# An attention step in another order: transposes in two groups between the scores, the output matmuls right ahead of the weighing

## What is computed

```
q: (4, 8, 1152, 64); k, v the same             # batch, heads, sequence, head size
q_pool = q.reshape(B, H, 576, 2, 64).mean(axis=3)
scores = scale * q_pool @ k^T                   # 576 x 1152 for each of 32 heads
attn   = exp(scores - max) / (sum + 1e-9)
x      = attn @ v, heads side by side           # (4, 576, 512)
logits = x @ w_gate                             # 8 experts; a ninth column, w_local, says "stay with
                                                # the expert of the token before"
out    = p[e] * (relu(x @ w1[e]) @ w2[e])       # one expert e for each token, 512 -> 1024 -> 512
```

## Time and profile before

| | |
|---|---|
| median of 3 runs | 824.21 us (821.65 to 826.23) |
| profiled execution | 825.53 us, span 823.7 us |
| busy | TensorE matmuls 98%, VectorE 55%, ScalarE 53%, GpSimd 45% |
| granted TensorE clock | 0.994 of full speed |
| attention | up to about 504 us; routing and experts after it |
| two middle phases, 13 and 14 | 30.08 us (first transposes at 201.16 us and at 231.24 us) |

### The profile page before, as it was taken

One profiled execution on the slowest core, in us unless ns is written; L12 is line 12 of the kernel. 1 busy time (PEld: TensorE's weight loads), 2 busy tenths in 40 slices (PEclk: granted clock), 3 DMA queues, 4 the chain that ended last, 5 costly groups with the idle time before them and its releaser, 6 DMA issues.

```text
span 823.7 us, 14479 instructions
## 1 busy us (share of the span) xinstructions
PE 806.9 (98%) x5291; PEld 528.5 (64%) x5292; DVE 453.4 (55%) x644; ACT 440.5 (53%) x876; POOL 366.6 (45%) x357
## 2 busy tenths in 40 slices
PE   7999999999999999999999999999999999999997
PEld 6787887878878778788788676633433433433432
DVE  6876776766757767767777555622332332332321
ACT  4776765866866767767667662224324324324321
POOL 5875666656647657557567512021221221221221
PEclk8999999999999999999999999999999999999999
DMA  7433243243243333344561005976615375010010
GB/s 242 162 124 97 83 160 99 63 156 102 71 146 101 84 134 93 115 126 127 187 210 45 15 1 154 327 251 229 229 47 184 109 257 184 27 45 20 31 45 20
DMA packets 52549, 100.94 MB, mean 123 GB/s; under 512 B 25406, under 2 KB 25936, under 8 KB 52499
## 3 DMA queue, kind: packets, MB, share of 16 engines
q1 hardware_dynamic: 48931, 90.03, 33.9%
q0 software_dynamic: 3568, 10.23, 3.6%
HBM read 90.78 MB, written 9.99 MB: 122 GB/s over the span
## 4 chain that ended last, share of the span: by engine, by line
PE 94%; DVE 3%; ACT 1%; DMA 1%; issue 0%; POOL 0%; SPq 0%; POOLq 0%; DVEq 0%
PE psum L599 15%; PE psum L638 15%; PE psum L1458 15%; PE psum L1480 15%; PE psum L669 13%; PE psum L626 4%; PE psum L705 2%; PE psum L653 2%; PE psum L1470 2%; PE psum L687 2%; PE psum L1393 2%; PE psum L673 2%; PE psum L1384 2%; PE psum L1446 1%; DVE negmax L983 1%; ACT probs L776 1%
## 5 line engine op out<-in xcount | busy, mean ns | idle before, releaser
L983 DVE TENSOR_REDUCE negmax<-psum 128x1 f32<-128x1152 f32 x144 | 195.4, 1358 | 64.0 <-PE psum L599 45.1
L599 PE MATMUL psum<-kstack,qstack 128*128 128x384 f32 x756 | 165.3, 354 | 0.2
L638 PE MATMUL psum<-ident,probs 128*128 128x128 f32 x1152 | 160.6, 275 | 2.1 <-DVE oT L997 1.2
L768 ACT ACTIVATE pT<-psum 128x512 f32<-128x512 f32 x192 | 114.9, 598 | 58.8 <-PE psum L638 56.8
L638 PEld LDWEIGHTS psum<-ident,probs 128*128 128x128 f32 x1152 | 134.9, 141 | 16.0 <-issue 6.2
L599 PEld LDWEIGHTS psum<-kstack,qstack 128*128 128x128 f32 x756 | 127.7, 190 | 0.9 <-ACT probs L776 0.9
L1460 PE MATMUL psum<-second,xgT 128*64 128x512 f32 x288 | 127.6, 595 | 0.0
L1458 PE MATMUL psum<-wbuf,xgT 128*64 x288 | 127.5, 595 | 0.0
L1480 PE MATMUL psum<-wbuf,shared 128*64 x288 | 126.6, 592 | 0.0
L1482 PE MATMUL psum<-second,shared 128*64 128x512 f32 x288 | 126.6, 592 | 0.0
L776 ACT ACTIVATE probs<-psum,negmax 128x768 f32<-128x768 f32 x128 | 115.7, 904 | 17.8 <-DVE negmax L983 17.4
(11 more groups left out here) (261 smaller groups left out, 1032.7 us busy)
## 6 DMA issues: line engine op xcount, KB each, us to landing
wbuf<-in_w SPq DMA_DIRECT2D x64, 512.0 KB
kraw<-in_k_t SPq DMA_DIRECT2D x32, 576.0 KB, 4.1
qraw<-in_q_t SPq DMA_DIRECT2D x31, 576.0 KB, 3.9
vraw<-in_v_t SPq DMA_DIRECT2D x16, 576.0 KB, 4.0
x_rows<-x_out SPq DMA_DIRECT2D x32, 128.0 KB
second<-in_w SPq DMA_DIRECT2D x8, 512.0 KB, 6.1
x_rows<-x_out SPq DMA_DIRECT2D x32, 16.0 KB
qraw<-in_q_t SPq DMA_DIRECT2D x1, 320.0 KB, 5.5
```

What stands on the lines that cost most here:

```text
L599: last = nc.tensor.matmul(dst[:, third, 0:THIRD], qstack[p % 2][:, part, tile_cols(side, i)], kstack[p % 2][:, side, third * THIRD:(third ...
L638: last = nc.tensor.transpose(dst[:, i * P:(i + 1) * P], probs[side][:, i, c * P:(c + 1) * P], ident[:])
L768: nc.scalar.activation(pT[:, c, :], bank(f, c), ACT.Copy).then_inc(bank_free(f, c), 1)
L983: nc.vector.tensor_reduce(negmax[:, p % 2, col:col + 1], slot(f, i)[:, :, 0:THIRD], AX.XY, ALU.max, negate=True).then_inc(max_ready, 1)
```

## The change

`out` moves from between t5 and s3 to right ahead of w, behind st or tt. t6 moves ahead of s3, so that s2 and s3 have two transposes (t5 t6) between them, as s0, s1 and s2 had; t7 and t8 stand together behind s3, ahead of st or tt. The copies follow: ScalarE now has t0, t1, t3, t5, t7 and VectorE t2, t4, t6, t8, so one copy a phase goes from ScalarE to VectorE. VectorE's scaling of `out` moves from between the maxima of s2 and s3 to behind the maximum of st or the copy of tt.

```diff
-OUT_AFTER = 5
-CODES_AFTER = 5
+OUT_AFTER = 8
+CODES_AFTER = 6
@@ TensorE
                 score(f, 2)
             if weighed(f):
                 turn(f, 5)
-            if projected(f):
-                output(f, "out", (2, 3) if f % 2 else (0, 1))
-            if f == LAST:
-                output(f, "out_last", (0, 1))
+                turn(f, 6)
             if scored(f):
                 score(f, 3)
...
             if weighed(f):
-                turn(f, 6)
                 turn(f, 7)
+                turn(f, 8)
             if scored(f) and f % 2:
                 score_tail(f)
             if weighed(f) and f % 2 == 0:
                 turn_tail(f)
+            if projected(f):
+                output(f, "out", (2, 3) if f % 2 else (0, 1))
+            if f == LAST:
+                output(f, "out_last", (0, 1))
             if weighed(f):
-                turn(f, 8)
                 weigh(f)
@@ ScalarE
             if weighed(f):
-                save_t(f, 6)
+                save_t(f, 7)
             if scored(f):
                 take_exp(f, 3)
-            if weighed(f):
-                save_t(f, 8)
             if scored(f) and f % 2:
                 take_exp_tail(f)
@@ VectorE
             if scored(f):
                 take_max(f, 2)
-            if projected(f):
-                output(f, "out", out_tiles(f))
-            if f == LAST:
-                output(f, "out_last", slice(0, FULL))
+            if weighed(f):
+                save_t(f, 6)
             if scored(f):
                 take_max(f, 3)
...
             if weighed(f):
-                save_t(f, 7)
+                save_t(f, 8)
             if scored(f) and f % 2:
                 take_max(f, "tail")
             if weighed(f) and f % 2 == 0:
                 save_tail(f)
+            if projected(f):
+                output(f, "out", out_tiles(f))
+            if f == LAST:
+                output(f, "out_last", slice(0, FULL))
             if weighed(f) and f % 2 == 0:
                 reciprocals(f)
```

## The result

| | before | after |
|---|---|---|
| median, 7 runs each on one chip | 826.11 us (821.65 to 826.48) | 829.85 us (828.79 to 830.23) |
| ratio | | 1.0055, interval 1.0041 to 1.0069 |
| profiled execution | 825.53 us, span 823.7 | 828.79 us, span 826.8 |

What follows compares the result with a forecast made beforehand. TensorE, with matmuls in work in 98% of the span, was taken as the bound. Middle phases 0, phase 25 +0.3 and the seam +2.4 gave +2.7 us on the 824.2 median, stated as 826.8 us, range 821 to 831.

Steps and rivals of the forecast that it cites:

- What bounds the kernel: Whole span: TensorE has work in 98%, so only its gaps or the chain between attention and experts can move the time.
- odd and even phases: TensorE's work in middle phases: odd saves 0.00 us, even 0.01, fifteen pairs 0, with 1.5 us each way.
- The joint ahead of w: Change to w's half-width matmuls: the 0.19 us loss stays with the change of width when `out` stands there.
- gain at the joints: Rival: the loss ahead of w vanishes behind `out`, 30 x 0.19 = 5.7 us less, 821.1 us; chance 0.12.
- Do the copies keep up?: Copies freeing banks for t7, t8 and `out` come out even, within 0.02 us; cost put at 0.
- copies slip: Rival: t7, t8 or s3 waits 0.15 us in each of 31 phases, +4.7 us, 831.5; chance 0.20.
- Moves with nothing behind them: Even phases: `x_out`, SyncE's queue and `add_logits` about 4 us later, covered by slack; otherwise up to 4 us, once.
- Phase 25: VectorE's `save_o` behind routing work: `x_out`'s 0.5 us comes ahead of it, less 0.25; +0.3 us, once.
- The seam: Phase 32, attention to experts: `x_out` 3.58 us later delays the second gather, so `add_halves(32)` starts 2.4 us later; bounds 0 to 3.6.
- The transfer's length: Second gather's landing: 3.4 us by the trace row, which the sum uses; 2.6 us by the skill, making the cost 1.6.
- Sum: Whole kernel: 0 + 0.3 + 2.4 = +2.7 us on a span of 823.7; from the median 824.2, 826.9, stated as 826.8.

Runs made afterwards that it cites:

- phases_only: Kernel after the change with the old order in phase 32 alone, phases 1 to 31 new; 824.38 us, ratio 1.0002 to the kernel before.
- warm: Kernel after plus 36 transposes of the identity on TensorE ahead of the last `out`, filling its wait; 834.65 us, ratio 1.0104 to the kernel before.
- gates_later: Kernel after with VectorE's one-time `projection_gates` moved from phase 1 to phase 2; 831.69 us, ratio 1.0074 to the kernel before.
- both_new: Kernel after with the gathers ahead of `add_logits` and `projection_gates` one phase later; 827.22 us, ratio 1.0025 to the kernel before.
- gather_first: Kernel after with phase 32's two gathers put ahead of `add_logits` in GpSimd's list; 825.24 us, ratio 1.0011 to the kernel before.
- scatter_first: Kernel after with phase 30's five scatters put ahead of `add_logits` in GpSimd's list, gathers unmoved; 827.88 us, ratio 1.0036 to the kernel before.
- seam_only: Kernel before with the new order in phase 32 alone; 830.32 us, ratio 1.0067 to the kernel before.
- both_old: Kernel before with the gathers ahead of `add_logits` and `projection_gates` one phase later; 823.46 us, ratio 0.9981 to the kernel before.

## Why the prediction was right, and where a size was off

The forecast was 826.8 us, in a range of 821 to 831, with "within 0.5%" as the likeliest. The kernel took 829.85, inside the range, and 0.55% over the kernel before, just beyond that bound (the interval of the ratio, 0.41 to 0.69%, has the bound in it). The likeliest of its three outcomes was thus narrowly missed, while the time, the direction and the reason for it came as it said.

- **What bounds the kernel; odd and even phases.** Right. 5.85 us from t5 to w as forecast, the pair unchanged at 30.08, and `phases_only` measures the thirty phases at 0.0 (1.0002, within 0.2% either way). In phase 14 the kernel after loads `out` at 225.28 and w at 225.97.
- **The joint ahead of w.** Right. In phase 13 `out` and the change to w take 212.14 - 211.21 = 0.93 us, where `out` alone took 0.71 ahead of s3: 0.22 go at the change, for the 0.19 that t8 had there. The rule of the Trainium skill, TensorEngine Tiling (Array Packing), Key Properties, that a change of tiling mode drains the engine, agrees with the trace: the loss stays with the change of width, whatever stands ahead of it. The drain itself no row shows. The rival "gain at the joints" falls.
- **Do the copies keep up?** Right. From 60 to 470 us the list of waits has one for TensorE's matmuls, 0.5 us for the codes' row in phase 20, which was 0.7 before. The margins of 0.02 us held. The rival "copies slip" falls.
- **Moves with nothing behind them.** Right for `x_out`, SyncE's queue and `add_logits` in the middle phases. One thing was missed here: behind `add_logits` in phase 30 stand the five scatters. They came later in the new order, and in `warm`, `gates_later` and `both_new` a halt of over 5 us ends with their landing; the kernel after was spared it.
- **Phase 25.** Too high: +0.3 forecast. `save_o` was late and the load of phase 26's t1 waited 0.18 us for it, but from t0 of phase 13 to t0 of phase 30 the kernel after takes 457.88 - 201.04 = 256.84 us and the kernel before 458.07 - 201.16 = 256.91, so the 0.3 did not stay.
- **The seam.** The mechanism was right link by link: `x_out` 496.60 - 487.94 = 8.66 us behind t0 of phase 32, where the working had 498.06 - 489.41 = 8.65, a DMA as `add_halves(32)`'s releaser, the wait of TensorE grown from 1.09 us, and `gather_first` takes it all back. The size was off, "+2.4 us" for 4.56. Of the 2.2 missing, 0.9 is the landing: the working took 3.4 us from the earlier trace rows, a median of two, and the second gather took 4.2. The other 1.25 is a term that the working did not have: TensorE came back from a wait of 4.22 us at half clock. The forecast had the wait ("from 1.1 to some 3.5 us") and did not ask what it does to the engine behind it.
- **The transfer's length.** The Trainium skill, DMA: Bandwidth & Descriptors, Anatomy of one DMA, gives by the estimate 2.6 us for 256 KB. The runs have 3.3 to 5.2 us from issue to landing for these indirect transfers, so the rows decide, against the page and against one value taken for all.
- **Sum.** On the spans 823.7 + 2.7 = 826.4 was forecast and 826.8 came, but by luck: 2.2 us more at the seam stand against 1.5 us that the kernel after is early at phase 32 (1.3 of it the halt that only the profile of before has) and the 0.3 of phase 25 that did not come. On medians the forecast was 3.05 us too low. 1.9 of that is the base: 824.21, from three runs, for the 826.11 of seven. The other 1.15 is the effect, 3.74 us for 2.6; by the means of the same runs it is 4.5, about what the seam costs in the traces.

Left open: why some builds halt between phases 30 and 31 and others don't, and whether the chip or the place of the scatters decides it.

## What to carry to other kernels

An instruction moved a few microseconds within a loop can be free thirty times and cost its full price once, in the last iteration, where the work that hid it has ended; look at what each in-order queue holds behind it there. An entry that doesn't need a late result goes ahead of the one that waits for it: here two entries moved in one list and a one-time step put off gave 0.3 to 0.4% together, more than the order of the matmuls. Where a change makes a wait of TensorE longer, price the matmuls behind the wait too: here waits of 3.6 to 4.7 us were followed by 0.8 to 2.1 us of extra time at the lower clock. And run a cure and what it is to cure on the same chip: here the halt of phase 31 can't be put down to the list, since the builds without it also ran elsewhere.

## What the runs showed of the hardware

- **Clock.** Behind waits of 1.09, 1.14 and 1.15 us the granted clock was 1.00. Behind 3.62, 3.75, 4.22 and 4.68 us it was 0.5 to 0.6 at first, and `out` to codes took 5.84, 7.09, 6.28 and 7.09 us for 5.03 (`scatter_first`, `seam_only`, the kernel after, `gates_later`): the cost does not follow the length of the wait. Behind 4.15 us of transposes of the identity in the place of the wait, it was 1.00.
- **Landing of an indirect transfer.** The same two gathers of 256 KB landed 3.3 to 5.2 us after issue in different builds.
- **A halt at a scatter's landing.** Engines that waited for nothing that the profile can name stood until the last of five indirect scatters had landed, TensorE for 1.0 us in the kernel before and in `both_old`, VectorE and ScalarE for over 5 us in `warm`, `gates_later` and `both_new`. In the four builds that issue them 4 to 10 us earlier it did not occur, nor in five that issue them late. Neither the cause nor what decides is shown.
- **Spread.** On the chip of `warm` the kernel before has two clusters of times: of 23 runs, 12 lie between 825.5 and 827.3 us and 11 between 822.3 and 824.4. What parts them was not found. Builds that are the same up to there differ by up to 2.7 us at w of phase 4 in their profiles (74.42 us in `phases_only`, 77.13 in `warm`).
